# Attention, channel mixing and routed experts in one kernel: the first stretch re-timed, the router's products turned round

## What is computed

```python
scores = scale * q @ k.T                        # 4 batches x 8 heads, 576 x 64
attn = exp(scores - max) where scores >= max - tau, else 0, over its row sum
x = attn @ v                                    # per batch 576 rows of 512
u = x + (x.T @ U @ V).T                         # token mixing of rank 32
x = u + relu(u @ w_ch1) @ w_ch2                 # 512 -> 2048 -> 512
logits = x @ w_gate;  local = sigmoid(x @ w_local)
e = argmax(logits[s]) if s == 0 or local < 0.5 else the expert of row s - 1
out[s] = softmax(logits[s])[e] * (relu(x[s] @ w1[e]) @ w2[e])   # 8 experts, 512 -> 1024 -> 512
```

## Time and profile before

| | us |
|---|---|
| median of 3 runs | 1185.02 (1183.88 to 1187.9) |
| the profiled execution | 1193.75 |
| its span | 1192.0 |
| of it, the first stretch and the passage behind it, to the end of the first token mixing | 129.4 |
| PE busy over the span | 1093.7 |

### The profile page before, as it was taken

How to read it: one execution, slowest core, us unless ns; L and a number is a source line. 1 busy time by engine, 2 the same in 40 slices (tenths; PEclk the granted TensorE clock), 3 DMA queues, 4 the chain that set the end, 5 groups by cost and what they waited for, 6 DMA issues and landing times. The chain is left out here.

```text
span 1192.0 us, 20141 instructions
## 1 busy us (share of the span) xinstructions
PE 1093.7 (92%) x7130; PEld 956.7 (80%) x7131; DVE 593.7 (50%) x1164; ACT 439.3 (37%) x730; POOL 347.3 (29%) x324
## 2 busy tenths in 40 slices
PE   6889899999989999998999989899947999999995
PEld 5566699898979989887998987799946887887784
DVE  4565555656455565645556552222257344255641
ACT  5465443333354333335333332211144244144530
POOL 4454005433411452341235314055011121121111
PEclk9898999999999999989999988999957999999998
DMA  6776115335161452415134112022057335154501
GB/s 152 177 188 156 30 27 140 96 94 141 53 152 42 125 130 81 120 60 145 41 105 113 69 36 94 18 72 71 1 198 267 123 123 186 37 189 143 206 32 37
DMA packets 110650, 127.28 MB, mean 107 GB/s; under 512 B 67213, under 2 KB 67213, under 8 KB 110544
## 3 DMA queue, kind: packets, MB, share of 16 engines
q1 hardware_dynamic: 104480, 114.54, 33.9%
q0 software_dynamic: 3520, 10.75, 2.8%
q10 hardware_dynamic: 2544, 0.59, 0.2%
HBM read 87.90 MB, written 10.22 MB: 82 GB/s over the span
## 5 line engine op out<-in xcount | busy, mean ns | idle before, releaser
L753 ACT ACTIVATE ex<-score_banks,stat 128x576 f32<-128x576 f32 x132 | 97.8, 741 | 199.6 <-DVE stat L857 199.6
L657 PE MATMUL mlp_banks<-u_hi,w_hi 128*128 128x320 f32 (+1 forms) x512 | 159.2, 311 | 12.4 <-DVE hid_lo L916 9.5
L665 PE MATMUL mlp_banks<-hid_hi,w_hi 128*128 128x320 f32 (+1 forms) x512 | 158.7, 310 | 7.6 <-DVE z L924 7.2
L462 POOL TENSOR_TENSOR w_lo<-stage,w_hi 128x1024 fp32r<-128x1024 f32 x64 | 152.5, 2383 | 4.6
L657 PE MATMUL mlp_banks<-u_hi,w_lo 128*128 128x320 f32 (+1 forms) x512 | 153.1, 299 | 0.0
L657 PE MATMUL mlp_banks<-u_lo,w_hi 128*128 128x320 f32 (+1 forms) x512 | 153.1, 299 | 0.0
L665 PE MATMUL mlp_banks<-hid_hi,w_lo 128*128 128x320 f32 (+1 forms) x512 | 152.5, 298 | 0.0
L665 PE MATMUL mlp_banks<-hid_lo,w_hi 128*128 128x320 f32 (+1 forms) x512 | 152.4, 298 | 0.0
L458 POOL CAST w_hi<-stage 128x1024 fp32r<-128x1024 f32 x64 | 66.5, 1039 | 273.7 <-PE mlp_banks L657 233.1
L867 DVE SCALAR_TENSOR_TENSOR ex<-score_banks,stat,ex 128x576 f32<-128x576 f32 x132 | 107.9, 817 | 58.2 <-ACT ex L753 50.2
L857 DVE TENSOR_REDUCE stat<-score_banks 128x1 f32<-128x576 f32 x132 | 99.4, 753 | 39.7 <-PE score_banks L590 30.3
(11 more groups left out here) (228 smaller groups left out, 2046.4 us busy)
## 6 DMA issues: line engine op xcount, KB each, us to landing
stage<-in_moe_w_ch SPq DMA_DIRECT2D x64, 512.0 KB, 3.9
w_raw<-in_moe_w SPq DMA_DIRECT2D x64, 512.0 KB, 5.4
q_tiles<-q_parts SPq DMA_DIRECT2D x30, 320.0 KB, 4.1
q_tiles<-q_parts SPq DMA_DIRECT2D x60, 160.0 KB, 4.3
k_tiles<-k_parts SPq DMA_DIRECT2D x60, 144.0 KB, 3.5
raw_q<-in_q SPq DMA_DIRECT2D x32, 128.0 KB, 3.0
raw_v<-in_v SPq DMA_DIRECT2D x32, 128.0 KB, 2.9
raw_k<-in_k SPq DMA_DIRECT2D x28, 128.0 KB, 2.9
```

Source lines behind the costliest of these rows:

```text
L462: nc.gpsimd.tensor_tensor(w_lo[:, n % RING], stage[:, n % 2], w_hi[:, n % RING].bitcast(F32), ALU.subtract).then_inc(w_split, 1)
L657: last = nc.tensor.matmul(bank[:, 0:w], ch1(a, g, d, c), of[:, d, cols], start=(d == 0 and n == 0), stop=(d == KC - 1 and n == 2))
L665: last = nc.tensor.matmul(bank[:, 0:w], ch2(a, g, q, c), of[:, q, 0:w], start=(q == 0 and n == 0), stop=(q == QUARTER - 1 and n == 2))
L753: nc.scalar.activation(ex_of(n), score_of(n), ACT.Exp, bias=stat[:, n % 4, 0:1], scale=-1.0).then_inc(exp_done, 1)
```

## The change

- **Values.** One chunk in each step, k = 0 at j = 4 to 8 and k = 1 at j = 0 to 3 of the next pair (two chunks at j = 2). The outputs are turned at j = 1 (k = 0) and j = 4 (k = 1), and `copy_out`, `inverse` and `write_x` move with them.
- **Parts of q and k.** Pair 2 is turned at j = 1, 2, 3 of pair 0, then pair p + 3 at j = 5, 6, 7 of pair p, all in the upper half of the bank `aux`. So five pairs are turned in the first stretch instead of four (`LATER`), and pair 6 no longer behind it; POOL's splitting and SP's stacking move to other steps, and pair 6 is still stacked in pair 5.
- **Pieces.** The first is split at step 15 instead of 9, the others at 17, 24, 26, 33, 35. SP issues the first two loads before the eight small transfers of U, and the loads of q and k of pair 3 before v of pair 1.
- **First passage.** At step 36 both outputs of pair 3 are turned, one on each side of `turn(36)`, and token mixing is put in step 37 instead of 38. All tasks of batch 0 come one task earlier or more.
- **Router.** A task `gate` takes the router weights as stationary, 32 columns wide (padded with zeros) for each quarter of z, in four column quarters of the array, and moves z of 256 or 320 columns; each quarter writes its own 32 partitions of the bank. ACT copies the result (`gate_part`), `logits` turns it, and DVE sums the four quarters. There are four tasks instead of two; at the second and third passage step 72 or 108 holds these four and the next step all five `rows`.

```diff
-LATER = PAIRS_OF + 2
+LATER = PAIRS_OF + 3
...
             tasks += [("channel", k, r, c) for c in range(KC)]
...
 NTASK = len(TASKS)
-TAIL = 2 + NT
-BY_ACT = [k in ("token_mix", "mixed", "hidden", "rows") for k, *_ in TASKS]
+TAIL = 4 + NT
+BY_ACT = [k in ("token_mix", "mixed", "hidden", "gate", "rows") for k, *_ in TASKS]
@@ -86,7 +87,9 @@
             plan.append([])
             continue
         ready = NTASK * b - (TAIL if at < ALONE else 0)
-        if at < 2:
+        if b == 1 and at < 2:
+            want = at
+        elif at < 2:
             ready = NTASK * (b - 1)
             want = 4 if at == 0 else TAIL
         elif at == 2:
...
-        first = (x // 2 + 1) * STEPS + 2 * (x % 2) if x < RING else STEP_OF[last_user(x)] + 1
+        first = (x // 2 + 1) * STEPS + 6 + 2 * (x % 2) if x < RING else STEP_OF[last_user(x)] + 1
...
     v4 = sb("v4", [P, S], F32R)
-    w_gate = sb("w_gate", [P, KC, E + 1])
+    w_gate = sb("w_gate", [P, KC, P // KC])
+    gate_part = sb("gate_part", [P, S])
...
-
-        order = ("q", "k", "tails") if p == 1 or p >= LATER else ("tails", "q", "k")
-        return parts_before(p) + order.index(part) + 1
+        return parts_before(p) + ("q", "k", "tails").index(part) + 1
 
     def part_bank(p, part):
-        at = 512 if part == "k" and p < LATER else 0
+        at = 512 if 2 <= p < LATER or (p == 1 and part == "k") else 0
         return aux[:, at:at + 512]
...
+        load_q_and_k(3)
         load_v(1)
...
-        load_q_and_k(3)
+        load_piece(0)
+        load_piece(1)
...
-        load_piece(0)
-        load_piece(1)
...
             if n < ALONE:
-                if j == 0 and p:
-                    stack_k(p + 1)
-                if j == 3 and p:
+                if p == 0 and j == 6:
+                    stack_q(2)
+                if p == 0 and j == 8:
+                    stack_k(2)
+                if p and j == 6:
+                    stack_q(p + 2)
+                if p and j == 7:
+                    stack_k(p + 2)
+                if p == 0 and j == 5:
+                    load_q_and_k(4)
+                if p and j == 0:
+                    load_q_and_k(p + 4)
+                if p and j == 4:
                     load_v(p + 1)
-                if j == 4 and p:
-                    load_q_and_k(p + 3)
-                if j == 6:
-                    stack_q(p + 2)
...
             else:
-                if p == PAIRS_OF and j == 0:
-                    stack_k(p + 1)
                 if j == 2 and p + 1 < PAIRS:
                     load_v(p + 1)
-                if j == 3 and p + 3 < PAIRS:
+                if j == 3 and PAIRS_OF < p and p + 3 < PAIRS:
                     load_q_and_k(p + 3)
-                if j == 4 and LATER <= p + 1 < PAIRS:
+                if j == 4 and LATER <= p + 2 and p + 1 < PAIRS:
                     stack_q(p + 1)
                     stack_k(p + 1)
...
-                if p and j == 6:
+                if p == 0 and j == 4:
+                    upper_q(2)
+                if p == 0 and j == 5:
+                    low_q(2)
+                if p == 0 and j == 6:
+                    upper_k(2)
+                if p == 0 and j == 7:
+                    low_k(2)
+                if p and j == 1:
                     spread_v(p - 1, n + 1)
-                if j == 4:
+                if p and j == 2:
                     upper_q(p + 2)
-                if j == 5:
+                if p and j == 3:
                     low_q(p + 2)
-                if j == 7:
+                if p and j == 4:
                     upper_k(p + 2)
-                if j == 8:
+                if p and j == 5:
                     low_k(p + 2)
-                for i in range(RING):
-                    if SPLIT_AT[i] == n:
-                        upper_piece(i)
-                    if SPLIT_AT[i] + 1 == n:
-                        low_piece(i)
...
-                if LATER <= p + 1 < PAIRS and j == 3:
+                if LATER <= p + 2 and p + 1 < PAIRS and j == 3:
...
+            for i in range(RING):
+                if SPLIT_AT[i] == n:
+                    upper_piece(i)
+                if SPLIT_AT[i] + 1 == n:
+                    low_piece(i)
@@ -538,17 +552,14 @@
             if p == 1:
...
-            elif p >= LATER:
-                if part == "q":
-                    pe.wait_ge(x_written, 2 * (p - 1) - 1)
-                else:
-                    pe.wait_ge(part_copied, part_count(p, part) - 1)
-            elif part == "q":
-                pe.wait_ge(part_copied, part_count(p, "tails"))
-            elif p == 2:
-                pe.wait_ge(part_copied, part_count(1, part))
+            elif part != "q":
+                pe.wait_ge(part_copied, part_count(p, part) - 1)
+            elif p < 4:
+                pe.wait_ge(part_copied, part_count(p - 1, "k" if p == 2 else "tails"))
+            elif p < LATER:
+                pe.wait_ge(x_written, 2 * (p - 3))
             else:
-                pe.wait_ge(x_written, 2 * (p - 2) - (1 if part == "tails" else 0))
...
             if 0 in chunks:
-                if p + 2 < LATER:
-                    pe.wait_ge(part_copied, part_count(p + 2, "k" if k else "q"))
-                elif k == 0 and LATER <= p + 1 < PAIRS:
+                if k and p + 3 < LATER:
+                    pe.wait_ge(part_copied, part_count(p + 3, "tails"))
+                if k == 0 and (p == 0 or LATER <= p + 1 < PAIRS):
                     pe.wait_ge(part_copied, part_count(p + 1, "tails"))
                 if p:
...
-            elif kind == "logits":
+            elif kind == "gate":
                 pe.wait_ge(loaded_gate, 32)
                 pe.wait_ge(dve_task, emptied(BY_DVE, b * NTASK + NTASK - TAIL - 1 - (1 - k) * (QUARTER + KC)))
+                for d in range(KC):
+                    last = nc.tensor.matmul(bank[d * (P // KC):(d + 1) * (P // KC), 0:w], w_gate[:, d], z_at(k, d, 0, w), start=True, stop=True)
+            elif kind == "logits":
                 for n, i in enumerate(range(*BLOCKS[k])):
-                    for d in range(KC):
-                        last = nc.tensor.matmul(bank[:, n * 16:n * 16 + E + 1], z_at(k, d, n * P, P), w_gate[:, d], start=(d == 0), stop=(d == KC - 1))
+                    first = START[k] + n * P
+                    last = nc.tensor.transpose(bank[0:ROWS[i], n * P:(n + 1) * P], gate_part[:, first:first + ROWS[i]], ident[:])
             else:
                 n = r - BLOCKS[k][0]
@@ -687,20 +701,18 @@
         for n in range(ALONE):
             p, j, _, _ = place(n)
             turn(n)
-            if p and j < 3:
-                values(p - 1, 1, ((0, 1), (2, 3), (4,))[j])
-            if j == 2:
-                turn_part(p + 2, "tails")
-            if p and j == 3:
+            if p and j < 4:
+                values(p - 1, 1, ((0,), (1,), (2, 3), (4,))[j])
+            if p and j == 1:
+                turn_out(p - 1, 0)
+            if p == 0 and 1 <= j < 4:
+                turn_part(2, ("q", "k", "tails")[j - 1])
+            if j >= 4:
+                values(p, 0, (j - 4,))
+            if p and j == 4:
                 turn_out(p - 1, 1)
-            if j == 3:
-                turn_part(p + 2, "q")
-            if 4 <= j < 7:
-                values(p, 0, ((0, 1), (2, 3), (4,))[j - 4])
-            if j == 6:
-                turn_part(p + 2, "k")
-            if j == 7:
-                turn_out(p, 0)
+            if 5 <= j < 8:
+                turn_part(p + 3, ("q", "k", "tails")[j - 5])
             if n + QUEUED < ALONE + 2:
                 pe.wait_ge(et_copied, n + 1)
                 scores(n + QUEUED)
...
-            if j == 1 and p <= PAIRS:
+            if n == ALONE:
+                turn_out(p - 1, 0)
+            elif j == 1 and p > PAIRS_OF and p <= PAIRS:
...
                 turn(n)
+            if n == ALONE:
+                turn_out(p - 1, 1)
             for t in fill[1:]:
...
+            elif kind == "gate":
+                nc.scalar.copy(gate_part[:, START[k]:START[k] + w], bank[:, 0:w]).then_inc(act_task, 1)
             elif kind == "rows":
@@ -813,15 +831,14 @@
             p, j, _, _ = place(n)
             copy_turned(n)
             exponentials(n + 2)
-            if p and j == 2:
+            if p == 0 and 1 <= j < 4:
+                copy_part(2, ("q", "k", "tails")[j - 1])
+            if p and j == 3:
                 copy_out(p - 1, 1)
-            if j == 2:
-                copy_part(p + 2, "tails")
-            if j == 3:
-                copy_part(p + 2, "q")
-            if j == 6:
+            if 5 <= j < 8:
+                copy_part(p + 3, ("q", "k", "tails")[j - 5])
+            if j == 8:
                 copy_out(p, 0)
-                copy_part(p + 2, "k")
         for n in range(ALONE, NSTEP):
             p, j, _, _ = place(n)
...
                 copy_out(p - 1, 1)
...
-                of = bank[:, 0:16 * (t1 - t0)].rearrange("p (t e) -> p t e", e=16)
```

(23 more changed lines are left out.)

11 lines of the change are left out of this document (7 added, 4 removed).

## The result

| | before | after |
|---|---|---|
| median, us | 1185.02 (7 runs, 1180.01 to 1190.41) | 1179.16 (7 runs, 1174.64 to 1180.42) |
| ratio | | 0.9936 (95%: 0.9908 to 0.9965) |
| the profiled execution | 1193.75 | 1179.56 |
| its span | 1192.0 | 1177.7 |

The change gains 5.9 us by the medians and 7.5 by the means (1185.9 and 1178.3), from which the ratio comes, of the 24 that were forecast. The two profiled executions are 14.2 us apart, more than the medians: that of before lies 8.7 us above its median, that of after on its own.

What follows compares the result with a forecast made beforehand. PE was taken as the bound, so time comes only from its gaps, removed work or clock. First stretch 8.7, first passage 5.0, pair 6's turnings 0.6 and router 10.0 made 24.3 us off the 1185.02 median: 1161, range 1148 to 1176.

Steps and rivals of the forecast that it cites:

- steps 9 to 17: First stretch: the weight-piece wait goes, PE stands about 2 us for the late stack before step 18's scores; 5.8 us less.
- reserve: First stretch: 2.0 us taken off the gain for turnings waiting for their mask and a fall or two of the clock.
- first passage: Steps 35 to 37, values, outputs and first token mixing: 18.1 us becomes 13.1, 5.0 less; 3.5 if mixing runs at half clock.
- both gates on PE: Router: both gates' products in four column quarters side by side take 1.2 us; one after the other 4.1.
- second, third, fourth passage to the end of the mixing: Router and token mixing at the later passages: second 0, third 1.5 us less, fourth 5.0 less.
- after the last batch: Last router, ahead of the expert program: 5.64 us becomes 2.4, rows a little quicker; 3.5 less, handed on whole.
- router in the medians: Router's whole term, summed over the later passages and the end of the last batch: 10.0 us less.
- Steps 18 to 34: First stretch, plain steps at 2.23 us: steps 18 to 26 1.7 us less, steps 27 to 34 2.2 less.
- My first rival: First stretch: the step does not shorten, DVE or ACT sets it at 2.5 us; 1165 us, chance 0.12.
- the second: Router: the gates' four quarters run in turn, losing 11 us of the gain; 1172 us, chance 0.12.
- The third: PE's clock stays up everywhere, so the reserve and half-clock mixings come back; 1154 us, chance 0.12.
- The fourth: Steps 0 to 35: slower, PE's clock goes to half and stays, about 0.45 us per us at half; up to 1205, chance 0.05.

Runs made afterwards that it cites:

- e3: The kernel before with only the router's change, the first stretch as it was: 1180.92 us, ratio to before 0.9955.
- e10: e7 with the router of before put back: 1169.80 us, ratio to before 0.9856.
- e13: e7 unchanged, run again on the same chip as e10: 1164.12 us, ratio to before 0.9805.
- e8: The changed kernel, SP's queue unaltered, with pair 3's queries and keys given their own buffers: 1166.74 us, ratio to before 0.9833.
- e1: The changed kernel with SP issuing pair 2's stack ahead of pair 4's load, and U's eight loads moved to pair 2: 1171.84 us, ratio to before 0.9888.
- e2: The changed kernel with only pair 4's load of queries and keys moved behind pair 2's stack on SP: 1174.40 us, ratio to before 0.9907.
- e6: e1 with the first two weight pieces and the three loads of v also moved behind the stack of pair 2's queries: 1166.61 us, ratio to before 0.9840.
- e7: e6 with DVE's two write_x of a step put behind its mask and minimum: 1163.10 us, ratio to before 0.9808.
- e4: The changed kernel with the router of before, so the first stretch's change alone: 1183.78 us, ratio to before 0.9978.

## Why the prediction was wrong

Forecast 1161 (1148 to 1176), measured 1179.2, outside the range. "Faster by more than 0.3%", given 0.92, holds. Step by step, in the profiled pair:

| step of the forecast | forecast, us | measured, us |
|---|---|---|
| steps 0 to 8 | -1.0 | -1.1 |
| steps 9 to 17 | -5.8 | **+4.3** |
| steps 18 to 26 | -1.7 | **+0.2** |
| steps 27 to 34 | -2.2 | -0.2 |
| reserve | +2.0 | in the rows above |
| first passage | -5.0, of it 11.6 long to the end of the mixing | 11.3 long to there |
| both gates on PE | 1.2 | 1.18 |
| ten turnings of pair 6; in the stretch from the first mixing to the second passage | -0.6 | -2.7 |
| second, third, fourth passage to the end of the mixing | 0, -1.5, -5.0 | -1.0, -2.8, -4.4 |
| after the last batch | -3.5 | -4.5 |
| stretches behind the second, third and fourth passage; expert program | 0; 0 | +1.8, -1.3, +0.8; +3.5 |
| router in the medians | -10.0 | -5.4 (e3), -5.7 (e10, e13) |

- **Steps 9 to 17: the step that failed.** "What is late next is SP" was right, and so was the stack's end (53.1 us forecast, 52.1 measured). Wrong was who waits for it first: "So PE stands for about 2 us", priced at the scores of step 18. The change moves POOL's split of pair 3 from step 13 to step 11, and that split waits for the same stack, with limit 12 behind it. I had counted POOL's moves as free ("POOL's other moves cost nothing") by its busy time and did not read its waits. e8 shows that this wait was the whole price of the late stack (12.4 us by the medians), e1, e2 and e6 that SP's order sets its length. The term is 10 us off; without the stall the kernel takes 1166.7, inside the range.
- **Steps 18 to 34.** The plain step came out at 2.15 us where I took 2.23. What took it back is the mask behind `write_x` on DVE, in two steps of each pair. The reserve named such waits, but 2.0 us were too little: they cost 3.9 up to the first mixing (e6 against e7). Without them a pair takes 21.4 us, where 21.0 was forecast. My first rival had this place ("a write of x beside one chunk") but called it DVE's work; it was its order.
- **First passage.** Right: 6.9 us from the turning of step 35 to the token mixing, where it had been 12.3. Of the stretch's gains it stayed, and so did one that the forecast did not have: about 3 us behind the first mixing, where PE's two longest waits became shorter and the clock no longer fell.
- **Router: right at its places, too large in the time.** The four places gained 12.7 us in the profiled pair and 10.6 between e4 and the changed kernel, where 10.0 were forecast; the medians gained 5.4 to 5.7. Two steps of the forecast stand behind that. It added up the places and put the stretches between them and the expert program at nothing ("handed on whole"), but 3.4 and 3.6 us of e4's 10.6 went back there: 0.8 through the fifth row copy, most of the rest where the clock fell at other places. And "I take the same 24.3 from it" took savings read in an execution 8.7 us above its median, part of them falls of its own: in e10, with a clock of 0.90 and 0.89, the third and fourth passage have only 1.0 and 2.3 us to win up to the mixing. e4's fourth passage, in an execution at its median, has 4.3. How the medians divide between the two is open.
- **Rivals.** The quarters ran side by side, so the second falls. They have all 128 rows in common, and yet their weight loads and products overlap: both gates take 1.18 us for sixteen instructions, against 4.1 worked out for one after the other. The Trainium skill (TensorE: Matmul & The Clock Gate, Part 3, The mechanism) says that a weight load overlaps a running matmul only where the row groups differ; this trace disagrees, and the measurement decides. That the products would then run in turn was my inference, and the page does not say it. The third came true in part: the falls at the passages went. It was worth nothing on top: the forecast had counted them already as savings, and other falls came in the stretches between. The fourth fell; half clock came behind the stall, for 10 us, as its result. Its price of 0.45 us for each us at half does not follow from the two pairs of rows named for it (1.45 of 6.01 and 1.68 of 4.59, both at half only in part). The first came true in part, since steps 18 to 34 gained nothing. The ends of the range lie 4 and 2.5 us beyond the sums named for them (1154 - 2.0 and 1172 + 1.5).

With the two orders mended the kernel takes 1163.1 and 1164.1 us, near the forecast. That the two waits were what kept the stretch from its gain is shown. That the total then comes within 3 us of 1161 is in part luck: the first mixing starts at 107.6 where 105 was forecast, the router gives 5.7 of 10, and the 3 us behind the first mixing were in no term. Why a fall of the clock comes in one execution and not in the next stays open; where it can come is in the last section.

## What to carry to other kernels

When an operation moves earlier, ask first for what it waits (here a single buffer still being copied out) and what stands behind it on its engine; busy time says nothing of that. Here a transfer's landing hung on what SP had issued ahead of it, so the transfer on which a compute queue waits goes before loads that nobody needs for a while. And savings at single places are not yet savings of the whole: follow them to the end of the span, and if the profiled execution lies above the median, work out which of its time the median has.
